# Three edits to a one-core attention, MLP and soft-expert kernel: two GEMM-1 blocks ahead of a data check, VectorE's first chunks in another order, and the last softmax in another order with filler matmuls

## The chip, the cores and the metric

The kernel runs on one core of a Trainium2 chip, as one launch. The metric is the time of the execution on the device in microseconds (us); lower is better. The time before is the median of three runs.

## The reference

Three layers in fp32. The first is a linear attention with a decay per feature, over 4 batches, 8 heads, 768 steps and head size 48. The second is an MLP on the 3072 x 384 result, with w_in (384 x 2048), a sigmoid gelu and w_out (2048 x 384). The third is a soft mixture of 8 experts with 4 slots each, d_ff 1024.

```python
for t in range(S):                      # attention
    cur = einsum('bhd,bhe->bhde', u[None] * kt, vt)
    y[:, :, t] = einsum('bhd,bhde->bhe', rt, state + cur)
    state = wt[:, :, :, None] * state + einsum('bhd,bhe->bhde', kt, vt)
h = x @ w_in                            # MLP
x = (h * (1.0 / (1.0 + exp(-1.702 * h)))) @ w_out
logits = x @ phi                        # 32 slots
d = softmax of logits over the 3072 tokens;  slot_input = d.T @ x
slot_out[e] = maximum(slot_input[e] @ w1[e], 0.0) @ w2[e]
c = softmax of logits over the 32 slots;     out = c @ slot_out
```

## The kernel before, in words

**Tiles and stages.** The sequence is cut into 24 chunks of 128 steps (`NCH`), and one chunk holds all eight heads of a batch. The MLP works in nine steps (`SIZES` = 2, 2, 2, 3, 3, 3, 3, 3, 3 chunks). In a step, GEMM-1 runs in 16 blocks of 128 hidden features (`F` counts the blocks over all steps, 0 to 143), each nine matmuls: every fp32 operand is split into a high and a low fp32r part, and three products are summed (xh·wi_hi, xl·wi_hi, xh·wi_lo). ScalarE takes the gelu of a block (L747) and rounds it to its high part (L751, `gh`). VectorE makes the low part (L1053, `gl`), and TensorE adds the block into GEMM-2 (L1241) two blocks later.

**What sets the order.** Each engine's program is written out by hand and walks one list, `slots_of_work`. An entry holds a block F, perhaps one of four pieces (j = 0 to 3) of a chunk's attention that this block hosts, perhaps a piece of the soft-expert softmax of the step before, and perhaps a job on the output softmax. Engines meet only at semaphores, so an instruction that waits holds all that stands behind it on its engine. In the first MLP step the attention of chunks 2 and 3 is hosted by blocks (2, 3, 5, 6) and (8, 9, 11, 12).

**The prologue.** Chunks 0 and 1 (`PRE` = 2) have no MLP work to host them. On VectorE `start_up()` (L966 to L1019) orders their pieces: `decays` and `invert` are scans over 516 elements; `decayed` and `grown_keys` make r and k for the score matmuls; `bonus` forms r·u·k by four instructions for each chunk (L867); `mask_scores`, `bonus_values` (bonus times v), `first_state` and `next_state` (the 48 x 48 states), `add_output`. On TensorE a chunk is `score` (L1145), four transposes (L1259), the bonus matmul (L1268), `gather_state` (L1156), `output` (L1165, L1171). TensorE then brings both outputs into the MLP's layout (`permute`, L1202, six fp32 matmuls of 128 columns each), ScalarE rounds them (`xh`, L794) and VectorE makes `xl` (L491). Between these stand matmuls on a zero tile (`keep_warm`, L1196).

**The data check.** The fast attention holds only if all decays lie in 0.625 to 1.5. Six slabs of 1536 columns are tested: slabs 0 to 2 on ScalarE (`test_decays`, L731 and L733), slabs 3 to 5 on VectorE (`bound_decays`, L963 and L964) and TensorE, which sums their bounds (L1304, L1306). A one-element matmul (L1312) and two VectorE instructions (L1003, L1004) give the flag. TensorE, VectorE and SyncE read it and branch. With these inputs the slow branch is not taken. Before, all of the MLP stands behind the branch.

**Weights.** w_in and w_out come in four slabs each through two staging buffers. ScalarE makes a slab's high part (`high_part`, L725), VectorE its low part (`low_part`, L1024), and only then does GpSimd issue the load of the slab after next. Counted through, even numbers are w_in, odd ones w_out.

**The tail.** After the last MLP step: three turns of x2 (L1352), logits (L1363), their maxima (L1100 to L1103), the exponentials (L817 to L819), the turn of e and l (L1370), the maximum over the three row groups (`common`, L1336 to L1338), `merge` (the normalised shares, with L1342), `add` (L1375, L1130), the slot inputs (L1384), ScalarE's copy `siT` (L465), and then the experts' first layer (L1394), relu (L462, L497), turns (L1406), second layer (L1425), and the output (L1450).

The lines on which the timing turns, in order: what VectorE does between the branch and the first blocks, how GEMM-2 waits, and the test's place on ScalarE.

```python
for j in range(4):
    front_part(PRE, j)      # decays, bonus, invert, decayed, grown_keys of chunk 2
low_part(1)
...
pe.wait_ge(gl_done, F - 1)  # GEMM-2 of block F - 2
...
early = {(0, 0): [(test_decays, 0)], (1, 0): [(high_part, 0), (test_decays, 1)],
         (1, 1): [(test_decays, 2)], (1, 3): [(high_part, 1)]}
```

## Time and profile before

| | |
|---|---|
| median of 3 runs | 626.76 us (626.35 to 627.07) |
| the profiled execution | 626.53 us, of which its span 624.8 us |
| mean granted TensorE clock | 0.978 |
| TensorE (PE) busy | 591.9 us, 95% of the span |
| VectorE (DVE) busy | 332.4 us, 53% |
| ScalarE (ACT) busy | 263.3 us, 42% |
| GpSimd (POOL) busy | 12.3 us, 2% |

The span is what the profile covers; the time of the execution is 1.73 us longer. The rows further below come from four views. The chain of waits is followed back from the last instruction, step by step, to what released it. The timeline lists instructions in order of time. The windows give the busy time of each engine in a stretch. The list of DMA issues gives size and time to landing. Overlapping instructions on TensorE are modelled, so a busy TensorE may still be a slow one: its granted clock (PEclk, 1.00 for 2.4 GHz and 0.50 for 1.2 GHz) stands beside it.

### The profile page before, as it was taken

How to read it: one execution, taken by the hardware profiler on the slowest of the kernel's cores; microseconds unless marked ns; L12 is line 12 of the kernel's file. 1: busy time of each engine (PE TensorE's matmuls, PEld its weight loads, DVE VectorE, ACT ScalarE, POOL GpSimd, SP SyncE). 2: the span in 40 equal slices, each digit the busy share in tenths (PEclk: the TensorE clock that was granted, in tenths of full speed). 3: DMA queues.
4: the chain of work that ended last, by engine and by line, in shares of the span. 5: the costliest groups of instructions: out<-in, count | busy, mean ns of one | idle time of the engine just before them, and what ended most of it. 6: DMA issues, size and time to landing. Idle time of an engine off the chain costs nothing.

```text
span 624.8 us, 15049 instructions
## 1 busy us (share of the span) xinstructions
PE 591.9 (95%) x6291; PEld 522.6 (84%) x6291; DVE 332.4 (53%) x730; ACT 263.3 (42%) x535; POOL 12.3 (2%) x30
## 2 busy tenths in 40 slices
PE   6969989999999999999999999999999999997983
PEld 4749889889989998999999989999999999995332
DVE  6879845648836662666356635664455324223214
ACT  3624634364353335433543354335433446453214
POOL 4001000000000000000000000000000000000000
PEclk9998999999999999999999999999999999998896
DMA  8937613204513331233123321233030196766528
GB/s 295 357 98 216 194 41 100 78 22 108 150 39 86 88 88 36 60 99 99 39 60 99 83 56 38 73 89 98 2 100 26 35 378 228 248 231 221 204 100 302
DMA packets 46309, 77.48 MB, mean 124 GB/s; under 512 B 3297, under 2 KB 35041, under 8 KB 43665
## 3 DMA queue, kind: packets, MB, share of 16 engines
q1 hardware_dynamic: 45040, 71.80, 37.1%
q0 software_dynamic: 1200, 4.72, 2.5%
q8 instruction: 50, 0.82, 0.6%
q14 instruction: 19, 0.15, 0.1%
HBM read 67.46 MB, written 9.04 MB: 122 GB/s over the span
## 4 chain that ended last, share of the span: by engine, by line
PE 90%; DVE 5%; issue 2%; POOL 1%; ACT 1%; DMA 1%; DVEq 0%; POOLq 0%; ACTq 0%
PE hps L1226 32%; PE acc L1241 32%; PE yps L1165 2%; PE mps L1259 2%; PE acc L1394 2%; PE zps L1145 2%; PE mps L1352 2%; PE zps L1165 2%; PE zps L1156 1%; PE zps L1171 1%; PE mps L1375 1%; PE mps L1363 1%; PE acc L1196 1%; PE mps L1425 1%; PE hps L1425 1%
## 5 line engine op out<-in xcount | busy, mean ns | idle before, releaser
L1053 DVE TENSOR_TENSOR gl<-g,gh 128x384 fp32r<-128x384 f32 (+1 forms) x144 | 73.9, 514 | 232.5 <-ACT gh L751 232.3
L1226 PE MATMUL hps<-xh,wi_hi 128*128 128x384 f32 (+1 forms) x432 | 147.2, 341 | 3.0 <-DVE xl L491 1.6
L1226 PE MATMUL hps<-xh,wi_lo 128*128 128x384 f32 (+1 forms) x432 | 137.2, 318 | 0.0
L1226 PE MATMUL hps<-xl,wi_hi 128*128 128x384 f32 (+1 forms) x432 | 137.1, 317 | 0.0
L1241 PE MATMUL acc<-wo_hi,gh 128*128 128x384 f32 x384 | 130.0, 338 | 4.2 <-DVE gl L1053 3.8
L1241 PE MATMUL acc<-wo_hi,gl 128*128 128x384 f32 x384 | 129.6, 338 | 0.0
L1241 PE MATMUL acc<-wo_lo,gh 128*128 128x384 f32 x384 | 129.6, 337 | 0.0
L747 ACT ACTIVATE g<-hps 128x384 f32<-128x384 f32 (+1 forms) x144 | 65.6, 456 | 142.0 <-PE hps L1226 138.4
L751 ACT ACTIVATE gh<-g 128x384 fp32r<-128x384 f32 (+1 forms) x144 | 70.4, 489 | 129.2 <-PE acc L1241 128.7
L1226 PEld LDWEIGHTS hps<-xh,wi_hi 128*128 128x128 f32 x432 | 81.4, 188 | 13.2 <-issue 8.3
L1226 PEld LDWEIGHTS hps<-xl,wi_hi 128*128 128x128 f32 x432 | 81.7, 189 | 0.9
L1226 PEld LDWEIGHTS hps<-xh,wi_lo 128*128 128x128 f32 x432 | 81.4, 188 | 0.0
L1241 PEld LDWEIGHTS acc<-wo_hi,gh 128*128 128x128 f32 x384 | 72.4, 188 | 5.5 <-DVE gl L1053 4.7
L1241 PEld LDWEIGHTS acc<-wo_lo,gh 128*128 128x128 f32 x384 | 72.5, 189 | 0.0
L1241 PEld LDWEIGHTS acc<-wo_hi,gl 128*128 128x128 f32 x384 | 72.4, 189 | 0.0
L860 DVE TENSOR_TENSOR_SCAN decay<-raw,restart 112x516 f32<-112x516 f32 x24 | 29.4, 1227 | 2.9 <-issue 1.6
L1165 PEld LDWEIGHTS yps<-rp,midway 48*48 48x48 f32 x384 | 22.9, 120 | 9.0 <-issue 5.2
L879 DVE TENSOR_TENSOR_SCAN inv<-raw,ends 112x516 f32<-112x516 f32 x24 | 29.6, 1234 | 0.8
L1165 PE MATMUL yps<-rp,midway 48*48 48x64 f32 x384 | 26.3, 218 | 2.9 <-DVE midway L931 2.8
L867 DVE SCALAR_TENSOR_TENSOR ruk<-raw,ucols 112x128 f32<-112x128 f32 x96 | 28.3, 337 | 0.0
L1165 PE MATMUL zps<-rp,state 48*48 48x64 f32 x384 | 25.9, 218 | 0.0
L1165 PEld LDWEIGHTS zps<-rp,state 48*48 48x48 f32 x384 | 22.4, 120 | 0.0
(225 smaller groups left out, 733.6 us busy)
## 6 DMA issues: line engine op xcount, KB each, us to landing
raw<-dmaj SPq DMA_DIRECT2D x23, 903.0 KB, 5.7
w1s<-w SPq DMA_DIRECT2D x16, 768.0 KB, 6.8
w2s<-w SPq DMA_DIRECT2D x16, 768.0 KB, 7.2
vn<-vnat SPq DMA_DIRECT2D x24, 192.0 KB, 2.5
tests<-wall SPq DMA_DIRECT2D x6, 768.0 KB, 14.0
out<-obuf SPq DMA_DIRECT2D x12, 384.0 KB, 4.1
y_scratch<-ybuf SPq DMA_DIRECT2D x44, 96.0 KB, 2.0
x<-y_scratch SPq DMA_DIRECT2D x22, 192.0 KB, 2.5
```

The lines of the kernel that those rows point to most:

```text
L747: act.activation(g32[F % 2][:, 0:wide], hps[F % 2][:, 0:wide], ACT.Gelu_apprx_sigmoid).then_inc(gelu_done, 1)
L751: act.activation(gh[F % 2][:, 0:wide], g32[F % 2][:, 0:wide], ACT.Copy).then_inc(gh_done, 1)
L860: dve.tensor_tensor_scan(flat[0], flat[1], flat[2], 1.0, ALU.mult, ALU.max).then_inc(scanned, 1)
L867: last = dve.scalar_tensor_tensor(ruk[n % 2][:, p, :], field(n, RR)[:, p], ucols[:, p:p + 1], field(n, KK)[:, p], ALU.mult, ALU.mult)
L879: dve.tensor_tensor_scan(flat[0][:, ::-1], later, flat[1][:, ::-1], 1.0, ALU.mult, ALU.add).then_inc(inverted, 1)
L1053: dve.tensor_tensor(out=gl[F % 2][:, 0:wide], in0=g32[F % 2][:, 0:wide], in1=gh[F % 2][:, 0:wide].bitcast(fp32), op=ALU.subtract).then_inc ...
L1145: last = pe.matmul(score_banks(n)[par][cols, p * HALF:(p + 1) * HALF], kd[n % 2][rows, p, cols], rp[n % 2][rows, p, cols], start=True, sto ...
L1165: return pe.matmul((zps, yps)[c][rows, p * HALF:(p + 1) * HALF], (state[n % 2], midway)[c][rows, p, :], rp[n % 2][rows, p, HALF * c:HALF * ...
L1226: last = pe.matmul(hps[F % 2][:, 0:wide], w[:, g, at:at + 128], v[i % 2][:, g, 0:wide], start=m == 0, stop=m == len(terms) - 1)
L1241: last = pe.matmul(acc[m][:, 0:DM], a[k][:, rows], w[:, f % CW, :], start=f == 0 and w is hi and a is gh, stop=f == NF - 1 and a is gl)
L1259: last = pe.transpose(mps[:, p * R:(p + 1) * R], kd[n % 2][:, p, :], ident[0:R, 0:R])
L1352: last = pe.transpose(ps[:, g * 128:(g + 1) * 128], x2[:, m, g * 128:(g + 1) * 128], ident[:, :])
```

## The change

**Prologue, checks.** ScalarE now tests four slabs (0, 1, 2, 4) and VectorE two (3, 5). ScalarE tests two of its four after it has made both `xh`. TensorE sums the bounds in pieces of 256 columns instead of 512.

**Prologue, GEMM-1.** Blocks 0 and 1 of GEMM-1 run ahead of the flag, between the sums. ScalarE's gelu of block 0 waits for `settled`, which one matmul behind TensorE's branch sets. On the slow branch both blocks are computed again.

**Prologue, order.** u is multiplied into four small head matrices (`heads_u`, by ScalarE), so that VectorE forms r·k in one instruction (`products`) and the bonus is four matmuls of 128 columns instead of one of 512. VectorE's pieces of chunks 0 and 1 stand in another order, `permute(0)` goes in front of `output(1)`, and chunk 2's front parts move from before `low_part(1)` to behind `gl` of blocks 0 and 1. In the first step the attention of chunks 2 and 3 is hosted by blocks (3, 4, 5, 6) and (8, 9, 10, 11). The load of phi is issued later.

**Tail.** For the last step only: e is turned before the maxima are combined, l is turned apart and later, and `add` comes before `merge`. The slot inputs are formed with unnormalised shares. The normaliser (one matmul against 128 columns, then `shares`) is applied as the scale of the experts' relu. Behind five groups of this stretch TensorE runs 2 to 4 fp32 matmuls of the identity with itself (`keep_ready`), 14 in all.

```diff
-TP, TA = 6, 3
+TP = 6
+ON_ACT, ON_DVE = (0, 1, 2, 4), (3, 5)
...
-SPAN = 512
+SPAN = 256
...
-                chunks = hosts[SIZES[i + 1]] if i else ((2, 3, 5, 6), (8, 9, 11, 12))
+                chunks = hosts[SIZES[i + 1]] if i else ((3, 4, 5, 6), (8, 9, 10, 11))
...
-                          for g in ("turn0", "turn1", "turn2", "logits", "common", "turn_e", "merge", "add")]
+                          for g in ("turn0", "turn1", "turn2", "logits", "turn_e", "common", "add", "merge")]
...
-                act.activation(hid[q][:, 0:512], (acc[0], acc[2])[q][:, :], ACT.Relu).then_inc(hid_act, 1)
+                act.wait_ge(merge_done, 1)
+                act.activation(hid[q][:, 0:512], (acc[0], acc[2])[q][:, :], ACT.Relu, scale=shares[:, 1:2]).then_inc(hid_act, 1)
...
-                dve.tensor_scalar(hid[q][:, 512:1024], (acc[1], hps[0])[q][:, :], 0.0, None, ALU.max).then_inc(hid_dve, 1)
+                dve.tensor_scalar(hid[q][:, 512:1024], (acc[1], hps[0])[q][:, :], shares[:, 1:2], 0.0, ALU.mult, ALU.max).then_inc(hid_dve, 1)
...
-            sp.dma_start(phis[:, :, :], phi.rearrange("(g p) s -> p g s", p=128)).then_inc(phi_in, 16)
...
+                    sp.dma_start(phis[:, :, :], phi.rearrange("(g p) s -> p g s", p=128)).then_inc(phi_in, 16)
                     sp.wait_ge(flag_made, 1)
...
+            def high_first(c):
+                act.wait_ge(permuted, c + 1)
+                act.activation(xh[0][:, :, c * C:(c + 1) * C], permuted_x(c), ACT.Copy).then_inc(xh_done, 1)
             early = {(0, 0): [(test_decays, 0)], (1, 0): [(high_part, 0), (test_decays, 1)],
-                     (1, 1): [(test_decays, 2)], (1, 3): [(high_part, 1)]}
+                     (1, 3): [(high_first, 0), (high_first, 1), (test_decays, 2), (test_decays, 3), (high_part, 1)]}
...
+            act.wait_ge(headsum_made, 1)
+            act.wait_ge(u_in, 16)
+            for p in range(HP):
+                last = act.activation(heads_u[:, p, :], headsum_f[:, :], ACT.Copy, scale=ucols[:, p:p + 1])
+            last.then_inc(heads_made, 1)
...
+                    if F == 0:
+                        act.wait_ge(settled, 1)
...
-                if F is None and attn == (PRE - 1, 3):
-                    for c in range(PRE):
-                        act.wait_ge(permuted, c + 1)
-                        act.activation(xh[0][:, :, c * C:(c + 1) * C], permuted_x(c), ACT.Copy).then_inc(xh_done, 1)
...
+                        act.wait_ge(l_turned, 1)
+                        act.activation(logits[:, BASE[i]:BASE[i] + SIZES[i], :],
+                                       acc[2][:, 0:NG].rearrange("t (a s) -> t a s", s=NS),
+                                       ACT.Copy).then_inc(el_done, 1)
...
+                        if i == NST - 1:
+                            act.activation(el[:, 0:wide], zps[:, 0:wide], ACT.Copy).then_inc(el_last, 1)
+                            continue
...
+            def products(n):
+                dve.tensor_tensor(out=ruk[n % 2][:, :, :], in0=field(n, RR), in1=field(n, KK), op=ALU.mult).then_inc(ruk_made, 1)
...
-                bonus(0, 0)
-                bonus(0, 1)
+                products(0)
+                dve.wait_ge(made, CONSTANTS)
+                for m in range(3):
+                    rows = slice(m * NS, (m + 1) * NS)
+                    dve.tensor_copy(fold[rows], ident[rows, rows])
                 decays(1)
-                dve.wait_ge(made, CONSTANTS)
                 mask_scores(0)
-                bonus_values(0)
                 invert(1)
+                decayed(1)
+                grown_keys(1)
                 first_state(0)
                 next_state(0)
-                decayed(1)
-                grown_keys(1)
-                bonus(1, 0)
+                bonus_values(0)
+                products(1)
                 add_output(0)
-                bonus(1, 1)
                 mask_scores(1)
                 bonus_values(1)
                 first_state(1)
                 next_state(1)
-                for m in range(3):
-                    rows = slice(m * NS, (m + 1) * NS)
-                    dve.tensor_copy(fold[rows], ident[rows, rows])
-                bound_decays(TA)
                 add_output(1)
                 low_part(0)
                 rest_x(dve, 0, 0)
                 rest_x(dve, 0, 1)
-                dve.wait_ge(tested, TA)
-                dve.tensor_reduce(outsum[:, :], outside[:, 0:TA], AX, ALU.add).then_inc(flag_sum, 1)
-                for k in range(TA + 1, TP):
-                    bound_decays(k)
+                for j in range(len(ON_DVE)):
+                    bound_decays(j)
+                dve.wait_ge(tested, len(ON_ACT))
+                dve.tensor_reduce(outsum[:, :], outside[:, :], AX, ALU.add).then_inc(flag_sum, 1)
...
-                for j in range(4):
-                    front_part(PRE, j)
...
+                if F in (0, 1):
+                    front_part(PRE, 2 * F)
+                    front_part(PRE, 2 * F + 1)
...
+                        dve.wait_ge(beta_done, 1)
+                        dve.tensor_scalar(merge[:, :, :], fold[:, :].unsqueeze(1).broadcast_to([NG, 4, NS]), beta[:, :], None,
+                                          ALU.mult).then_inc(den_weighted, 1)
...
-                        dve.wait_ge(beta_done, 1)
-                        dve.wait_ge(den_done, NST)
-                        chain(dve.tensor_scalar(merge[:, 0, :], fold[:, :], beta[:, :], None, ALU.mult))
-                        dve.tensor_scalar(merge[:, 1, :], merge[:, 0, :], den[:, NST % 2:NST % 2 + 1], None,
-                                          ALU.mult).then_inc(den_weighted, 1)
                         dve.wait_ge(den_merged, 1)
-                        chain(dve.tensor_scalar(merge[:, 2, :], zps[0:NG, 0:NS], 1e-9, None, ALU.add))
-                        chain(dve.reciprocal(merge[:, 2, :], merge[:, 2, :]))
-                        dve.tensor_tensor(out=merge[:, 1, :], in0=merge[:, 0, :], in1=merge[:, 2, :],
-                                          op=ALU.mult).then_inc(merge_done, 1)
+                        chain(dve.tensor_scalar(shares[:, 0:1], yps[:, 0:1], 1e-9, None, ALU.add))
+                        dve.reciprocal(shares[:, 1:2], shares[:, 0:1]).then_inc(merge_done, 1)
...
+            def keep_ready(times):
+                for _ in range(times):
+                    pe.matmul(hps[1][:, 0:128], ident[:, :], ident[:, :], start=True, stop=True)
...
+                        pe.wait_ge(heads_made, 1)
                         pe.wait_ge(ruk_made, n + 1)
-                        pe.matmul(bonus_bank(n)[0:R, :], headsum_f[:, :], ruk[n % 2][:, :, :].rearrange("d p t -> d (p t)"),
-                                  start=True, stop=True).then_inc(u_done, 1)
+                        for p in range(HP):
+                            last = pe.matmul(bonus_bank(n)[0:R, p * C:(p + 1) * C], heads_u[:, p, :], ruk[n % 2][:, p, :],
+                                             start=True, stop=True)
+                        last.then_inc(u_done, 1)
...
+                if F is None and attn == (PRE - 1, 2):
+                    pe.wait_ge(y_done, 1)
+                    pe.wait_ge(scored, 2 * PRE)
+                    permute(0, permuted)
                 if F is None and attn == (PRE - 1, 3):
-                    for c in range(PRE):
-                        pe.wait_ge(y_done, c + 1)
-                        permute(c, permuted)
-                        keep_warm(WARM)
+                    pe.wait_ge(y_done, PRE)
+                    permute(1, permuted)
+                    keep_warm(WARM)
+                    pe.wait_ge(xl_done, PRE)
+                    pe.wait_ge(lo_done, 1)
+                    hidden_layer(0).then_inc(h_done, 1)
                     pe.wait_ge(ones_made, 1)
-                    for k in range(TA, TP):
-                        pe.wait_ge(bounded_done, k - TA + 1)
...
-                        last.then_inc(bounds_summed, 1)
-                        if k + 1 < TP:
-                            keep_warm(WARM)
+                    sum_bounds(0)
+                    hidden_layer(1).then_inc(h_done, 1)
+                    sum_bounds(1)
                     pe.wait_ge(flag_sum, 1)
...
+                    pe.matmul(acc[0][:, 0:256], warm[:, 0:128], warm[:, 128:384], start=True, stop=True).then_inc(settled, 1)
...
+                    elif what == "turn_e" and i == NST - 1:
+                        pe.wait_ge(et_done, NST)
...
+                        pe.wait_ge(e_done, NST)
+                        pe.transpose(acc[2][:, 0:NG], lT[:, :], ident[0:NG, 0:NG]).then_inc(l_turned, 1)
                     if what == "merge":
+                        pe.wait_ge(gathered_done, NST)
                         pe.wait_ge(den_weighted, 1)
-                        pe.matmul(zps[0:NG, 0:NS], ones_sq[:, :], merge[:, 1, :], start=True, stop=True).then_inc(den_merged, 1)
+                        for g in range(G):
+                            last = pe.matmul(mps[:, g * NS:(g + 1) * NS], gathered[:, g * 128:(g + 1) * 128], merge[:, 0, :],
+                                             start=True, stop=True)
+                        last.then_inc(si_psum, 1)
+                        pe.wait_ge(den_done, NST)
+                        pe.matmul(yps[:, 0:1], merge[:, :, :].rearrange("r a s -> r (a s)"), den[:, NST % 2:NST % 2 + 1],
+                                  start=True, stop=True).then_inc(den_merged, 1)
+                        keep_ready(3)
...
+                        if ends and m == 2:
+                            keep_ready(3)
...
+                        if i == NST - 1:
+                            pe.transpose(zps[:, 0:wide], eT[0:wide, :], ident[0:wide, 0:wide]).then_inc(e_turned, 1)
+                            keep_ready(2)
...
-            pe.wait_ge(*mps_read)
-            pe.wait_ge(gathered_done, NST)
-            pe.wait_ge(merge_done, 1)
-            for g in range(G):
-                last = pe.matmul(mps[:, g * NS:(g + 1) * NS], gathered[:, g * 128:(g + 1) * 128], merge[:, 1, :],
-                                 start=True, stop=True)
-            last.then_inc(si_psum, 1)
```

On VectorE, from the flag to the first score mask of chunk 2, the order before is the following. `wo_lo` and `wi_lo` are the low parts of weight slabs, `gl` those of MLP blocks, `decay`, `ruk`, `inv`, `rp`, `kd` chunk 2's front parts.

```order
L860 SCALAR_TENSOR_TENSOR decay_71<-raw_67,restart 112x516
L867 SCALAR_TENSOR_TENSOR ruk_79<-raw_67,ucols 112x128 x2
L875 RECIPROCAL ends<-decay_71 112x4
L879 SCALAR_TENSOR_TENSOR inv<-raw_67,ends 112x516
L867 SCALAR_TENSOR_TENSOR ruk_79<-raw_67,ucols 112x128 x2
L885 TENSOR_TENSOR rp_75<-raw_67,decay_71 112x512
L890 TENSOR_TENSOR kd_77<-raw_67,inv 112x512
L1024 TENSOR_TENSOR wo_lo_58<-stage_119,wo_hi_57 128x1536
L1053 TENSOR_TENSOR gl_110<-g_0_105,gh_107 128x256
L1024 TENSOR_TENSOR wi_lo_52<-stage_118,wi_hi_51 128x1536
L1053 TENSOR_TENSOR gl_111<-g_1_106,gh_108 128x256
L1053 TENSOR_TENSOR gl_110<-g_0_105,gh_107 128x256
```

In the changed kernel the same place on VectorE reads:

```order
L1048 TENSOR_TENSOR wo_lo_58<-stage_120,wo_hi_57 128x1536
L1076 TENSOR_TENSOR gl_111<-g_0_106,gh_108 128x256
L884 SCALAR_TENSOR_TENSOR decay_71<-raw_67,restart 112x516
L891 SCALAR_TENSOR_TENSOR ruk_79<-raw_67,ucols 112x128 x2
L903 RECIPROCAL ends<-decay_71 112x4
L907 SCALAR_TENSOR_TENSOR inv<-raw_67,ends 112x516
L891 SCALAR_TENSOR_TENSOR ruk_79<-raw_67,ucols 112x128 x2
L1048 TENSOR_TENSOR wi_lo_52<-stage_119,wi_hi_51 128x1536
L1076 TENSOR_TENSOR gl_112<-g_1_107,gh_109 128x256
L913 TENSOR_TENSOR rp_75<-raw_67,decay_71 112x512
L918 TENSOR_TENSOR kd_77<-raw_67,inv 112x512
L1076 TENSOR_TENSOR gl_111<-g_0_106,gh_108 128x256
```

The low part of the w_out slab and of block 0 now come first, and `kd` of chunk 2 stands behind four more instructions than it did.

On TensorE, the tail from the last logits to the first expert matmul reads before:

```order
L1363 MATMUL mps<-x2t,phis 32x128 x9
L1336 MATMUL yps<-ident,top 1x96
L1338 MATMUL yps<-ones,common 96x1
L1370 MATMUL mps<-ident,eT 128x96
L1370 MATMUL mps<-ident,lT 128x96
L1342 MATMUL zps<-merge,ones_sq 96x32
L1375 MATMUL mps<-x_112,el 32x384 x3
L1384 MATMUL mps<-merge,gathered 128x32 x3
```

and after, where `hps<-ident` rows are the fillers:

```order
L1422 MATMUL mps<-x2t,phis 32x128 x9
L1218 MATMUL hps<-ident 128x128 x4
L1431 MATMUL zps<-ident,eT 128x96
L1218 MATMUL hps<-ident 128x128 x2
L1383 MATMUL yps<-ident,top 1x96
L1385 MATMUL yps<-ones,common 96x1
L1388 MATMUL acc<-ident,lT 128x96
L1442 MATMUL mps<-x_113,el 32x384 x3
L1218 MATMUL hps<-ident 128x128 x2
L1393 MATMUL mps<-merge,gathered 128x32 x3
L1397 MATMUL yps<-den,merge 128x1
L1218 MATMUL hps<-ident 128x128 x3
```

The turn of e stands ahead of the maxima now, the normaliser's matmul behind the slot inputs, and fillers stand between, three of them directly ahead of the experts.

## Rows read from the trace of the kernel before

**Rows 1.** Page, the chain that ended last: its shares by engine.

```profile
PE 90%; DVE 5%; issue 2%; POOL 1%; ACT 1%; DMA 1%; DVEq 0%; POOLq 0%; ACTq 0%
```

**Rows 2.** Chain of waits, prologue and first step: start us, us, what.

```profile
26.66 1.34 PE hps L1202 x12
...
37.34 0.15 DVE flag L1004
...
45.96 2.29 PE acc L1241 x6
...
88.42 1.33 PE hps L1226 x9
```

**Rows 3.** Timeline, VectorE: start us, us, instruction, [idle before <-releaser].

```profile
25.96 0.95 DVE L964 TENSOR_SCALAR bounded<-tests 128x1536 fp32r<-128x1536 f32 x1
...
36.63 0.68 DVE L1003 TENSOR_REDUCE insum<-acc 1x1 f32<-1x512 f32 x1 [2.04 <-PE acc L1312]
...
39.10 1.23 DVE L860 TENSOR_TENSOR_SCAN decay<-raw,restart 112x516 f32<-112x516 f32 x1 [1.62 <-issue]
...
48.80 0.43 DVE L1053 TENSOR_TENSOR gl<-g,gh 128x256 fp32r<-128x256 f32 x1 [0.89 <-ACT gh L751]
...
65.43 1.76 DVE L1024 TENSOR_TENSOR wo_lo<-stage,wo_hi 128x1536 fp32r<-128x1536 f32 x1 [2.87 <-ACT wo_hi L725]
...
80.76 0.41 DVE L954 TENSOR_TENSOR ybuf<-yps,ybuf 112x256 f32<-112x256 f32 x1
```

**Rows 4.** Timeline, ScalarE, 25 to 64 us.

```profile
25.61 1.56 ACT L731 ACTIVATE tests<-tests,test_bias 128x1536 f32<-128x1536 f32 x1
...
28.68 0.18 ACT L733 ACTIVATION_READ_ACCUMULATOR tests<-tests,test_bias 128x1 f32 x1
...
29.96 0.49 ACT L794 ACTIVATE xh<-hps 128x384 fp32r<-128x384 f32 x1 [0.72 <-PE hps L1202]
...
40.11 0.39 ACT L747 ACTIVATE g<-hps 128x256 f32<-128x256 f32 x1 [8.28 <-PE hps L1226]
...
63.91 1.49 ACT L725 ACTIVATE wo_hi<-stage 128x1536 fp32r<-128x1536 f32 x1 [3.15 <-DMA stage<-w_out]
```

**Rows 5.** Timeline, TensorE, 17 to 20 us.

```profile
17.03 0.22 PE L1165 MATMUL yps<-rp,midway 48*48 48x64 f32 x1 [0.95 <-DVE midway L931]
...
19.92 0.60 PE L1259 MATMUL mps<-ident,kd 112*128 112x112 f32 x4
```

**Rows 6.** DMA issues of 45 to 46.5 us: median us to landing last.

```profile
stage<-w_out POOLq DMA_DIRECT2D x1, 768.0 KB, 5.0
```

**Rows 7.** DMA issues of 54 to 55 us.

```profile
stage<-w_out POOLq DMA_DIRECT2D x1, 768.0 KB, 9.4
```

**Rows 8.** Windows: stretch, length, busy us of PE, PEld, DVE, ACT, POOL, PEclk, DMA, GB/s.

```profile
44.00:46.00 2.00, 0.04 (x1) 0.04 (x1) 2.00 (x3) 0.00 (x0) 0.12 (x1) 0.57 0.00 0
...
573.00:574.00 1.00, 0.54 (x5) 0.48 (x8) 0.37 (x2) 0.25 (x2) 0.00 (x0) 0.67 0.87 326
...
583.00:584.00 1.00, 1.00 (x12) 0.32 (x8) 0.00 (x0) 0.60 (x1) 0.00 (x0) 0.71 0.00 0
```

**Rows 9.** Chain of waits, tail: start us, us, what.

```profile
560.56 0.78 PE mps L1375 x6
...
569.63 0.89 PE mps L1363 x18
...
571.33 0.26 PE yps L1336
...
573.99 1.47 PE mps L1375 x6
...
576.19 1.47 PE mps L1384 x6
...
577.99 8.11 PE acc L1394 x48
...
586.53 2.71 PE acc L1394 x24
```

More of the change, by code:

```diff
@@ L129, in attention_mlp_soft_experts @@
             xl[i] = sb(f"xl{i}", [128, G, ST], f32r)
+        heads_u = sb("heads_u", [R, HP, R], at=place[0])
         g32 = [sb(f"g32_{i}", [128, ST]) for i in range(2)]
@@ L862, in bonus @@
             def bonus(n, half):
-                if n == 0 and half == 0:
+                if n == PRE and half == 0:
                     dve.wait_ge(u_in, 16)
@@ L1322, in _ @@
                         pe.wait_ge(split_again, PRE)
+                        for F0 in range(2):
+                            hidden_layer(F0)
+                    pe.matmul(acc[0][:, 0:256], warm[:, 0:128], warm[:, 128:384], start=True, stop=True).then_inc(settled, 1)
                 if job is not None and job != "exps":
```

105 lines of the change are left out of this document (61 added, 44 removed).

## The prediction

> **What bounds the kernel now.** I read the chain of waits first. TensorE carries 90% of it, VectorE 5% [rows 1], so most of the span is matmul work that the change leaves alone. What can move are the places where TensorE isn't the bound, and the chain has two: the prologue with the first MLP step, and the tail between the last MLP block and the experts.
>
> In the prologue the flag is started at 37.34, and TensorE's next link of weight is GEMM-2 of block 0 at 45.96 [rows 2]. Between them stand VectorE's branch (1.62 us of "issue"), chunk 2's front parts from 39.10, and `low_part(1)`; ScalarE had its first gelu at 40.11 [rows 3, 4]. From 39.10 to the end of chunk 3's output (80.76 + 0.41 = 81.2) VectorE waits only twice for any length: 0.89 us for a gelu and 2.87 us for ScalarE, which itself waited 3.15 us for a w_out slab [rows 3, 4]. So the stretch is VectorE's, and the first block of the second step starts at 88.42 [rows 2]. In the windows the granted clock falls to the lower level (1.2 GHz) in 44 to 46, after TensorE stood idle [rows 8].
>
> In the tail the chain hops between engines from 569.63 to 577.99 [rows 9]. The clock falls in 573 to 574 (mean 0.67) and is back in 583 to 584 (0.71) [rows 8]: it is low from about 573.3 to 583.4, 10.1 us.
>
> **The change part by part: up to the flag.** (1) VectorE's order. TensorE waited 0.95 us for `midway` of chunk 0 at 17.03 [rows 5], because the scan `inv` stood ahead of it. Now the state comes as soon as its matmuls are through, and chunk 1 starts up to 0.95 us earlier; I take 0.75, since `keep_warm` matmuls stand in the gap. (2) `permute(0)` (1.34 us [rows 2]) moves ahead of `output(1)` and stays on the path, but the group of `keep_warm` behind it goes: about 0.6. The second `xh` was at 29.96 [rows 4]; 29.96 - 0.75 - 0.6 = 28.6, over at 29.1.
>
> (3) The bonus is four matmuls of 128 columns with a load each, in place of one of 512. Four transposes with four loads took 0.60 [rows 5], and a `permute` matmul of 128 columns 1.34 / 6 = 0.22. So the split costs between 0 and 0.9 a chunk; I take 0.1, the row with four loads. The Trainium skill (TensorE: Matmul & The Clock Gate, section Step-by-step: what each phase is for) says that weight loads are pulled ahead of running matmuls; by that the split costs nothing, and the sum would be 0.1 better. (4) `heads_u` is four small copies on ScalarE, and `products` one instruction for four on VectorE: both lie beside the wait for GpSimd's constants.
>
> (5) The tests. A slab took ScalarE from 25.61 to 28.86, and 3.17 where one follows another [rows 4]. Two now stand behind the second `xh`: 29.1 + 6.35 = 35.45. VectorE's two slabs are at most four times 0.95 [rows 3] behind `xl`, about 33.5, and TensorE, with two GEMM-1 blocks and 24 short sums in between, also comes out near 35.3: all three engines meet. With the sum of 0.15 and the one-element matmul the reduction starts near 35.8, not 36.63, and takes 256 elements in place of 512: near 0.42 (a 256-column instruction on VectorE takes that [rows 3]) instead of 0.68. The flag comes 0.85 + 0.25 = **1.1 us earlier**. No idle slot is left on ScalarE there: what it is late, the flag is late.
>
> (6) The load of phi, now issued at about 27 us, isn't needed before the second step: nothing.
>
> **From the flag to block 16.** The branch costs what it cost (1.62). `low_part(1)` and `gl` of block 0 are done at 39.6 and 40.0 instead of 45.6 and 45.9, because 4.8 us of front parts stand behind them now, and because ScalarE has its gelu at about 38.0, right behind `settled`, not at 40.11. But VectorE has the same instructions in both orders, and it is the bound, so the gain isn't these 6 us. It is the flag's 1.1, plus what VectorE no longer waits. Of 3.76 us (0.89 + 2.87) I count:
> - GpSimd loads a slab when `low_part` of the slab before it in its buffer is done. `low_part(1)` six us earlier starts slab 3 at 40. Alone it takes 5.0 [rows 6], and VectorE reaches `low_part(3)` at about 47. It ends at 48.8 instead of 54.2, and slab 5, issued at 49, takes 9.4 at worst [rows 7]. It is there at 58.5, and VectorE, by its own queue, gets to `low_part(5)` at 60.7. The 2.87 goes.
> - The 0.89 goes too, since gelu and `gh` of block 2 are done at about 41.8.
> - What is late next: near 63 VectorE waits for TensorE's block 7 and 8, which can't run faster than about 2.1 us a block. I make that wait 1.65.
>
> So 3.76 - 1.65 = 2.1, and **the first step ends 1.1 + 2.1 = 3.2 us earlier**: block 16 at 85.2 instead of 88.4. TensorE's own idle stretch (42.2 to 45.6, for `gl` of block 1, behind the scans) stays, and so, I expect, does the fall of its clock in it. This costs little, since VectorE is the bound there. Later steps run as before.
>
> **The tail.** What the low level costs is in the rows: `add` takes 1.47 against 0.78 for the same six records at full clock, the slot inputs 1.47 (0.78 by the same ratio), and the first 48 expert matmuls 8.11 against 2 x 2.71 [rows 9]: 0.69 + 0.69 + 2.69 = 4.1 us.
>
> A filler is an fp32 matmul of 128 columns: 0.22 by `permute` [rows 2], 0.15 by the transposes [rows 5]. I take 0.22, the plain matmul. The Trainium skill (TensorE: Matmul & The Clock Gate, section Terms) gives fp32 a transpose mode four times as fast, by which the transposes' row would make a filler 0.60, and the tail 2.4 us longer than I sum. The `permute` row speaks against that.
>
> With the clock kept: four fillers behind the logits end at 571.4, under the wait for the exponential; e is turned at 571.8; two fillers later TensorE turns the maxima at 572.4, not 571.33 (+1.1). Maxima, spread and the turn of l take it to 573.8, `add` to 574.6, VectorE's accumulation to 575.3, the slot inputs to 576.05, the normaliser's matmul and three fillers to 577.0. Experts start at 577.0, not 577.99: -1.0. (ScalarE's `siT`, 0.3, lies under the fillers; the two fillers behind `add` under VectorE.) With 2.69 for the experts, **the tail is 3.7 us shorter**. The scale in the relu costs nothing: `shares` are ready two us before.
>
> **Sum.** 626.53 - 3.2 - 3.7 = 619.6 for the profiled execution. The median lies 0.2 above its time: **619.9 us**.
>
> **Rivals.**
> - *A: the clock isn't kept in the tail* (624.3). For it: it fell in the middle of small matmuls, at one waiting about 0.6 to 0.8 us at each hop, and hops stay. Against it: TensorE would be occupied some 80% of 569.6 to 577, where now it is half of that. Then `add` and the slot inputs lose 1.4, the last four small groups and fillers about 1.0, and the experts start at 579.4; if the clock is back at 583.4 as now, they lose 2.0. End of these 24 + 24 matmuls: 586.8, against 586.1 now: +0.7, so 626.53 - 3.2 + 0.7 + 0.2.
> - *B: the slabs still set the first step* (622.0). VectorE's 2.87 stays, or another wait takes its place, if slab 3 takes 9.4 as slab 5 did, since its high part stands ahead of a gelu on ScalarE. Then only the flag's 1.1 is left: 626.53 - 1.1 - 3.7 + 0.2. For it: 9.4 [rows 7]; against it: 5.0 when alone [rows 6], and nothing else is loaded at 40.
> - *C, slower: TensorE's clock doesn't come back in the first step* (629.8). It falls in the idle stretch before 45.6, and the work behind it is broken up by waits for VectorE. A microsecond of dense work at the lower level costs half a microsecond (8.11 against 5.42 [rows 9]). If it stays low for 20 us more than now, that is +10, and 619.9 + 9.9 = 629.8. It decides from 14 us (6.9 / 0.5). Against it: the same dip is there now, and ends within seven us.
> - *D: nothing to be seen* (626.8): ScalarE's tests come so late that the flag isn't earlier, and the fillers eat what the clock gives back.
>
> **How the numbers follow.** The forecast has 0.60, A 0.14, B 0.16, C 0.05, D 0.05. A and B are faster too, so faster by over 0.2% (1.25 us, about what a measurement of this kernel tells from no change) has 0.90, within it 0.05, slower 0.05. The open costs are the bonus (up to 0.8 more a chunk), the fillers (0.5 less to 2.4 more) and VectorE's waits (2.1 less to 1.7 more). The range takes in A and B, and leaves out C, D and the far ends: 618.0 to 624.6.
>
> **What would show it.** In the profile after: the flag near 36.2, first gelu near 38.0, GEMM-2 of block 0 near 40.1; no wait of ScalarE for a w_out slab near 60; block 16 near 85.2. In the tail, PEclk 1.00 throughout, `add` near 0.8, and the first 48 expert matmuls in 5.4. Wrong: a flag at 37 or later; VectorE waiting over 2 us for a high part; PEclk 0.50 behind the logits; a last block of the first step that starts no earlier than before.

## The result, and the profile after

| kernel | median, us | executions | range | ratio to before, 95% interval |
|---|---|---|---|---|
| before | 627.0 | 80 (all jobs) | 623.8 to 630.3 | |
| changed | 623.65 | 7 | 620.3 to 625.8 | 0.9947, 0.9921 to 0.9973 |
| changed, all three jobs | 622.1 | 19 | 620.1 to 625.8 | 0.9947, 0.9910 and 0.9920 |

A job is one session in which executions of the changed kernel and of the kernel before were timed side by side. The change makes the kernel faster, by 3.1 us in the first job and by 4.9 over all executions. I had forecast 6.9. The executions of the changed kernel spread over 5.7 us, so 1.5 of the 3.8 us missing in the first job is its median's place in that spread. The profiled execution took 622.08, its span 620.4 against 624.8: 4.4 less. The page's shares of the chain are like those of before [rows 1]:

```profile
PE 88%; DVE 5%; issue 2%; DMA 2%; POOL 1%; ACT 1%; DVEq 0%; SPq 0%; POOLq 0%; ACTq 0%
```

The chain of waits in the prologue and the first step answers to [rows 2] (start us, us, what):

```profile
12.60 1.71 PE acc L1311 x8
...
22.34 0.47 issue
...
37.26 0.15 DVE flag L1030
...
46.62 2.29 PE acc L1283 x6
...
53.78 0.43 ACT gh L771
...
80.22 3.39 DMA y_scratch<-ybuf
...
83.77 2.44 DMA x<-y_scratch
...
```

The flag (the instruction on VectorE that ends the data check) starts 0.08 us earlier than before, where I had put 1.1. GEMM-2 of block 1 (2.29 for its six matmuls) runs at the lower clock, which I call half clock below. A piece called `issue` on TensorE is a rest for which the profile shows no cause. The end of the first step is no longer a matmul chain but chunk 3's way through memory: its store, then the load of x.

VectorE's timeline answers to [rows 3]:

```profile
36.81 0.41 DVE L1029 TENSOR_REDUCE insum<-acc 1x1 f32<-1x256 f32 x1 [0.28 <-PE acc L1354]
...
38.95 1.76 DVE L1048 TENSOR_TENSOR wo_lo<-stage,wo_hi 128x1536 fp32r<-128x1536 f32 x1 [1.55 <-issue]
...
54.24 0.43 DVE L1076 TENSOR_TENSOR gl<-g,gh 128x256 fp32r<-128x256 f32 x1 [1.20 <-ACT gh L771]
...
66.40 0.42 DVE L1076 TENSOR_TENSOR gl<-g,gh 128x256 fp32r<-128x256 f32 x1 [1.68 <-ACT gh L771]
```

The reduction over 256 elements takes 0.41 (0.68 before), as forecast. The waits of 2.87 and 0.89 are gone and 1.68 has come near 66 (I had 1.65), but 1.20 at 54.24 is new: the `gh` it waits for hangs on GEMM-1's block 4, which TensorE ran at half clock. ScalarE's timeline, with [rows 4]:

```profile
25.54 0.49 ACT L747 ACTIVATE xh<-hps 128x384 fp32r<-128x384 f32 x1 [0.31 <-PE hps L1253]
29.50 0.49 ACT L747 ACTIVATE xh<-hps 128x384 fp32r<-128x384 f32 x1 [3.48 <-PE hps L1253]
...
39.29 0.38 ACT L767 ACTIVATE g<-hps 128x256 f32<-128x256 f32 x1 [1.58 <-PE acc L1367]
```

The second `xh` comes at 29.50 instead of my 28.6, and ScalarE stands idle for 3.48 us ahead of it. The windows, with [rows 8] (stretch, length, busy time of PE, PEld, DVE, ACT, POOL, PEclk, DMA share, GB/s):

```profile
9.00:16.00 7.00, 6.57 (x87) 6.14 (x88) 5.19 (x11) 3.67 (x4) 0.24 (x2) 0.59 1.03 408
...
44.00:52.00 8.00, 5.38 (x48) 4.83 (x49) 8.00 (x14) 3.23 (x5) 1.51 (x2) 0.59 0.54 179
84.00:92.00 8.00, 6.05 (x72) 5.42 (x71) 3.00 (x8) 3.20 (x8) 0.00 (x0) 1.00 0.08 25
560.00:577.00 17.00, 16.06 (x125) 13.09 (x126) 6.49 (x19) 6.08 (x17) 0.00 (x0) 1.00 0.69 234
577.00:600.00 23.00, 22.98 (x228) 8.22 (x224) 4.60 (x9) 4.86 (x9) 0.00 (x0) 1.00 0.60 207
```

From 9 to 16 us the clock is at the lower level (mean 0.59). For the profiled execution of before the same window shows 1.00, but the durations there say otherwise. Set beside e9, the kernel before with a longer warm-up (below), its first matmuls take as long as at half clock. In the chain of before, and then in that of e9:

```profile
9.84 1.13 PE hps L1145 x32
10.97 0.94 PE mps L1259 x4
...
13.00 1.22 PE acc L1268 x2
```

```profile
9.67 0.69 PE hps L1145 x32
10.37 0.53 PE mps L1259 x4
...
11.50 0.87 PE acc L1268 x2
```

The changed kernel's first two groups are the same as before's (1.13 and 0.94). Half clock lasted to about 13.7 in before's execution (0.35 us more than 0.87 is some 0.7 us at half clock) and to 14.7 here. So both profiles have the half clock in the prologue, here for one us more. The tail's chain, with [rows 9]:

```profile
567.91 0.67 PE hps L1218 x6
568.58 0.87 PE mps L1422 x18
571.05 0.47 PE hps L1218 x4
572.78 0.81 PE mps L1442 x6
...
574.28 0.85 PE mps L1393 x6
575.33 0.78 PE hps L1218 x6
576.11 5.29 PE acc L1455 x48
```

The groups `hps L1218` are the fillers. `add` takes 0.81 instead of 1.47, the slot inputs 0.85 instead of 1.47, the first 48 expert matmuls 5.29 instead of 8.11. Block 16 started 1.0 us earlier than before, the outputs' first matmul 4.47 (604.17 against 608.64): the tail gave about 3.4 of the 4.4 us, prologue and first step 1.0.

### The profile page after: what moved, and what is told of

The parts are those of the page before. It is cut to its first block, busy times and chain, and to the rows that moved or that the text cites. A ratio compares the mean times of both kernels' runs of the same rounds, so it can differ in the third digit from the quotient of the medians.

```text
span 620.4 us, 15118 instructions
## 1 busy us (share of the span) xinstructions
PE 589.9 (95%) x6326; PEld 527.6 (85%) x6326; DVE 329.1 (53%) x719; ACT 267.9 (43%) x542; POOL 12.6 (2%) x30
## 4 chain that ended last, share of the span: by engine, by line
PE 88%; DVE 5%; issue 2%; DMA 2%; POOL 1%; ACT 1%; DVEq 0%; SPq 0%; POOLq 0%; ACTq 0%
PE hps L1233 32%; PE acc L1283 31%; PE yps L1187 2%; PE mps L1301 2%; PE zps L1167 2%; PE mps L1409 2%; PE zps L1178 2%; PE zps L1187 2%; PE zps L1193 1%; PE acc L1455 1%; PE mps L1422 1%; PE mps L1442 1%; PE hps L1486 1%; PE acc L1223 1%; PE mps L1486 1%
## 5 line engine op out<-in xcount | busy, mean ns | idle before, releaser
L891 DVE SCALAR_TENSOR_TENSOR ruk<-raw,ucols 112x128 f32<-112x128 f32 x88 | 25.9, 336 | 0.0
```

Source lines behind the costliest of these rows:

```text
L891: last = dve.scalar_tensor_tensor(ruk[n % 2][:, p, :], field(n, RR)[:, p], ucols[:, p:p + 1], field(n, KK)[:, p], ALU.mult, ALU.mult)
```

## The experiments

Each was timed in five rounds beside the kernel before. The runs e5a to e8a have the edits and expectations of e5 to e8, which gave no time. Line numbers are those of the kernel in question. "Flag" is the start of that instruction on VectorE, "block 16" that of the second step's first matmul, both in the profiled execution, as is the span. Bonus(0) is the bonus matmul of chunk 0. All times are in us.

| run | median (n) | ratio, 95% | flag | block 16 | span |
|---|---|---|---|---|---|
| before | | | 37.34 | 88.42 | 624.8 |
| changed | 623.65 (7) | 0.9921 to 0.9973 | 37.26 | 87.40 | 620.4 |
| e4 changed again | 621.17 (6) | 0.9883 to 0.9936 | 35.65 | 84.93 | 619.5 |
| e12 changed, third | 622.05 (6) | 0.9900 to 0.9939 | 36.26 | 86.79 | 619.9 |
| e1 tail alone | 624.85 (12) | 0.9944 to 0.9973 | 37.67 | 90.48 | 623.8 |
| e2 front alone | 625.80 (12) | 0.9960 to 0.9991 | 37.38 | 87.93 | 624.3 |
| e3 no fillers in the tail | 624.54 (10) | 0.9936 to 0.9968 | 36.95 | 85.83 | 623.2 |
| e5a test between | 620.92 (7) | 0.9879 to 0.9941 | 35.92 | 84.95 | 621.4 |
| e6a rests filled | 619.39 (6) | 0.9850 to 0.9909 | 35.24 | 83.70 | 617.0 |
| e7a longer warm-up | 620.36 (6) | 0.9854 to 0.9915 | 35.29 | 84.16 | 618.9 |
| e13 the same again | 620.83 (6) | 0.9888 to 0.9945 | 35.10 | 83.54 | 616.6 |
| e14 first step's rests | 620.85 (6) | 0.9871 to 0.9913 | 37.65 | 86.33 | 619.8 |
| e8a blocks behind flag | 623.98 (12) | 0.9930 to 0.9973 | 36.06 | 87.54 | 620.6 |
| e9 before, longer warm-up | 626.45 (12) | 0.9970 to 1.0000 | 37.84 | 88.87 | 623.8 |
| e10 e5a and e6a | 619.57 (5) | 0.9846 to 0.9889 | 38.53 | 86.97 | 619.9 |
| e11 and chunk 3 earlier | 619.32 (5) | 0.9859 to 0.9900 | 34.34 | 82.78 | 615.6 |

**The two halves.** e1 has only the tail's hunks of the diff, e2 only the others.

> The kernel before with the tail's part of the change alone (order of the last step's softmax, row sums merged into the experts' scale, filler matmuls). Theory 1 (the two parts of the change add up; the tail gave 3.4 of the 4.4 us by which the span shrank): 626.8 - 3.4 = 623.4, ratio 0.9946, the 48 first expert matmuls in 5.3 to 5.5 us and the block at slot 16 still at 88.4. Theory 2 (the parts depend on each other, because the clock in the tail follows what the whole kernel did before): 625 to 627.

> The prologue's part of the change alone, with the tail of the kernel before. Theory 1: 626.8 - 1.0 = 625.8, ratio 0.9984, block 16 at 87.4, the expert matmuls 8.1 us again. Rival (the prologue's part is worth nothing by itself and its 1.0 us is one execution's scatter): 626.8. What I had predicted for it was 623.6.

The tail alone gives 2.1 us (ratio 0.9959), the front alone 1.2 (0.9975); together 3.3 by the medians and 4.1 by the ratios, the whole change 4.9 by the medians of all jobs: as well as these intervals can tell, they add up. Of my two terms the front's 3.2 is far off, and the tail's 3.7 lies just outside e1's interval (1.7 to 3.5). One profile can mislead here: up to block 16, e1 does the work of before, and in its profile block 16 comes 2.06 us later than in that of before, with the rest of the span 3.06 shorter.

**The tail's fillers.** e3:

```
             def keep_ready(times):
-                for _ in range(times):
-                    pe.matmul(hps[1][:, 0:128], ident[:, :], ident[:, :], start=True, stop=True)
+                for _ in range(0):
+                    pass
```

> The changed kernel without its 14 filler matmuls in the tail; all else of the tail's reordering stays. Theory 1 (the fillers keep the granted clock at 1.00 there, as the reordering alone does not): the clock falls in the tail, the 48 first expert matmuls take 8.1 instead of 5.3 us, the six adds 1.47 instead of 0.81, time 623.65 + 3.2 = 626.8. Rival (the shorter chain between the matmuls keeps the clock by itself): 623.3 to 623.7, since the fillers cost at most 0.3.

2.4 us slower than the changed kernel (622.1), where I had expected 3.2. The clock falls to a mean of 0.84 in 560 to 577, and the chain has the low-clock durations back:

```profile
572.51 1.47 PE mps L1442 x6
...
576.53 7.97 PE acc L1455 x48
```

So the fillers are what keeps the clock. From e2 (old tail) to e3 the reordering alone gives 1.3 us, from e3 to the changed kernel the fillers 2.4. They don't keep it every time: of twelve profiled kernels with fillers, two (e5a and e7a) show means of 0.92 and 0.90 in 560 to 577, and e7a's 48 expert matmuls took 6.13.

**The changed kernel again** (e4, e12).

> The changed kernel once more, unchanged, to see which differences between the two profiled executions come back. Theory 1: median 623.0 to 624.3, ratio 0.9947; in the profile the flag at 37.3, gelu(0) at 39.3, the idle 1.2 us of VectorE before the difference of tile 4, block 16 at 87.4, the experts' 48 matmuls in 5.3. Rival (the first step's 1.0 us is scatter): block 16 anywhere from 86.5 to 88.4, and the median elsewhere with it.

> The changed kernel a third time, beside the next two on one chip. Theory 1 (its time is the sum of a fixed part and of stretches at half clock and fetch rests in the prologue, which differ from execution to execution): median 622.3, executions from 620 to 626, span minus the flag's start 583.1 to 583.9 as in its two profiles.

The two profiles of one kernel, e4 here beside the one above, differ by 1.6 us at the flag. In e4 the chain and the windows read:

```profile
12.56 1.12 PE acc L1311 x8
...
84.93 2.29 PE hps L1233 x9
```

```profile
9.00:16.00 7.00, 6.43 (x99) 5.70 (x101) 5.97 (x14) 3.68 (x4) 0.24 (x2) 0.76 1.04 408
...
44.00:52.00 8.00, 6.66 (x71) 5.94 (x72) 8.00 (x15) 5.73 (x9) 1.51 (x2) 1.00 0.48 165
84.00:92.00 8.00, 7.07 (x67) 6.73 (x68) 3.32 (x7) 2.54 (x6) 0.00 (x0) 0.79 0.00 0
```

By the windows the low clock ended near 13.0 instead of 14.7, bonus(0) took 1.12 instead of 1.71, and there was no `issue` rest of 0.47 at 22.3. TensorE's rest before GEMM-2's block 1 was nearly as long (2.71 against 3.15) and the clock stayed at 1.00 behind it; it fell in the rest before block 16 instead (2.42 us), whose matmuls then took 2.29 instead of 1.31. So where the half clock falls changes from one execution to the next, and not by the length of the last rest alone: in e12 it fell ahead of GEMM-2's block 1 too, behind rests of only 1.53 and 1.37. In e12 the span less the flag's start is 583.6, close to the other two (583.1 and 583.9): what the flag is late, the end is late.

**Filling TensorE's rests** (e6a all three, e7a and e13 the warm-up, e14 the first step's two).

```
-WARM_UP = (512,) * 8
+WARM_UP = (512,) * 18
...
+                    if F == NF:
+                        pe.wait_ge(y_done, BASE[2])
+                        keep_busy(8)
...
+                    if F == 3:
+                        keep_busy(12)
                     pe.wait_ge(gl_done, F - 1)
```

> The changed kernel with matmuls on zeros in three rests of TensorE: 10 more of 512 columns in the warm-up (it rests there from 5.2 to 9.4), 12 of 256 columns ahead of GEMM-2's block 1 (rest 43.5 to 46.6) and 8 ahead of block 16 (rest 85.2 to 87.4). Theory 1 (the missing 2 us and the scatter of 5.7 us between executions are stretches at half clock that follow these rests): granted clock 1.00 from 2 to 95 us, bonus(0) in 1.12 instead of 1.71 us, GEMM-2 block 1 in 1.05 instead of 2.29, time 622.3 - 0.9 (prologue) - 1.0 (first step) = 620.4 and the spread under 3 us. Rival (half clock comes back in another rest, or the fillers push the work behind them): 622 to 623.

> The changed kernel with the longer warm-up alone (18 matmuls of 512 columns instead of 8). Theory 1: clock 1.00 from 9.4 to 15 us, flag 0.9 us earlier than in executions at half clock there (37.3 to 36.4 or less), time 622.3 - 0.9 = 621.4; the first step's own stretch at half clock stays. Rival (the constants or the loads of v set the start of the prologue and nothing is gained): 622.3.

> The changed kernel with the longer warm-up alone, again (18 matmuls of 512 columns instead of 8). Theory 1 (half clock in the prologue costs the changed kernel 1.5 to 2 us and cost the kernel before 0.3 to 0.7): 620.4, ratio 0.988 to 0.990, that is 1.9 under the changed kernel. Rival (the 1.9 us between 620.36 and 622.27 came from different chips and sessions): the same median as the changed kernel in this job, within 0.5.

> The changed kernel with the fillers in the first step alone (12 ahead of GEMM-2's block 1, 8 ahead of block 16), the warm-up as it was. Theory 1 (the first step's half clock costs 1.0, whether it falls on GEMM-2's block 1 or on block 16): 622.3 - 1.0 = 621.3, flag as in the changed kernel, block 16 within 48.5 us of the flag instead of 49.3 to 50.1. Rival (the clock of the first step follows from the prologue's, and without the longer warm-up the fillers do nothing): 622.3.

By the medians the warm-up is worth 1.5 us (12 executions, median 620.6, against 19 of the changed kernel, 622.1), the first step's fillers 1.3, all three 2.7. The scatter of the times isn't gone with it: 1.9 us over e6a's six executions, but 7.3 over e13's six and 4.0 over the five each of e10 and e11, so those stretches of half clock aren't its only source. In the direct comparison of e12 and e13 the warm-up gave 1.2, with overlapping intervals, so its size is known to perhaps one us; the flag is better evidence. With the clock at 1.00 from 9 to 16 us it starts at 35.10 to 35.29, in three profiles out of three; with bonus(0) at half clock (1.59 to 1.71) it starts at 36.3 to 37.7, in five (changed, e2, e3, e12, e14). In e14 the flag is late, and block 16 still comes 48.7 us behind it. But that isn't shown to be the fillers' work: in its profile the half clock fell at 40 to 44, ahead of them, as it did in e3, which has no such fillers and 48.9. Their worth rests on the times, whose intervals overlap with the changed kernel's. The windows of e13:

```profile
9.00:16.00 7.00, 5.44 (x121) 4.79 (x124) 6.44 (x15) 3.79 (x4) 0.24 (x2) 1.00 1.03 407
38.00:44.00 6.00, 4.56 (x23) 3.85 (x21) 5.97 (x11) 3.03 (x6) 0.77 (x1) 0.72 0.47 140
44.00:52.00 8.00, 7.21 (x74) 6.32 (x74) 7.97 (x17) 5.65 (x9) 1.51 (x2) 1.00 0.57 191
```

My expectation for e6a, 1.00 throughout, was wrong. The clock falls in 38 to 44 there too (0.77), with all three rests filled, as it does here in e13: soon after TensorE's rest at the branch (1.25). It costs little at that place, since block 16 follows the flag by 48.4 to 48.5 in both.

**The same warm-up in the kernel before** (e9; the same edit of `WARM_UP`).

> The kernel before with the longer warm-up alone. Theory 1 (before the change TensorE had slack in the prologue, so its half clock cost little there: flag at 37.67 with it in the run with the tail's edits, 37.34 without; the change took the slack away, so that the same half clock costs 1.2 to 2 us): flag at 37.3, time 626.8 - 0.3 = 626.5, ratio 0.9995. Rival (the half clock costs both kernels alike, and the profiled execution of before had merely escaped it): ratio 0.997, as the changed kernel gained 1.9 us of its 622.3 by this warm-up.

The ratio is 0.9985 (0.9970 to 1.0000): 0.7 us, between the two theories' 0.3 and 1.9. The flag doesn't come earlier at all: 37.84, with bonus(0) in 0.87, against 37.67 in e1, where it took 1.71. Theory 1 would explain that by TensorE's slack in the prologue (the 0.95 of [rows 5]), which would have taken up the half clock. The chain of e9 speaks against it:

```profile
16.73 0.78 PE acc L1196 x4
...
25.11 1.34 PE hps L1202 x12
...
28.27 1.95 issue
30.21 0.28 PE hps L1202
```

TensorE still waits 0.94 for `midway`, and yet it is 1.8 us ahead of before's profile at the first of these rows (18.57 there) and 1.55 ahead at `permute(0)` (26.66). The slack had hidden little of the half clock. The lead went in a rest of 1.95 in the middle of `permute(1)`, which before's profile doesn't have. Without it, by my estimate (30.52 - 1.95), the second `xh` would have started at about 28.6, which is 1.4 ahead of before's. The changed kernel, for its part, waits for `midway` again when its clock is up (1.1 us in e6a, e7a and e13), and its chunk 1 starts no earlier than e9's: 17.41 to 17.59 against 17.44. So the half clock reaches `permute` in both kernels. Whether the kernel before gains less from the warm-up than the changed one stays open: the interval of e9 goes from 0 to 1.9 us and holds both theories.

**The flag earlier** (e5a).

```
-  (1, 3): [(high_first, 0), (high_first, 1), (test_decays, 2), ...
+  (1, 3): [(high_first, 0), (test_decays, 2), (high_first, 1), ...
...
                     sum_bounds(0)
-                    hidden_layer(1).then_inc(h_done, 1)
                     sum_bounds(1)
...
                               skip_group_check=True).then_inc(flag_psum, 1)
-                    keep_warm(WARM)
+                    hidden_layer(1).then_inc(h_done, 1)
```

> The changed kernel with ScalarE's third decay test between the two rounded copies of x (in the 3.48 us in which ScalarE idles there) and GEMM-1's block 1 behind the flag's sums on TensorE. Theory 1 (the flag waits for the four tests and for TensorE's sums, which end together): both end 1.1 us earlier, flag at 36.1 instead of 37.3 in an execution with the same clock, block 16 as much earlier, time 622.3 (the changed kernel's median over both sessions) - 1.1 = 621.2. Rival (a first step that is set by VectorE's chain from flag to chunk 3 keeps nothing of it, since slabs and x loads keep their own dates): 622.3. Second rival: the test delays the second rounded copy and with it VectorE's remainder by 0.2 to 0.5, and the flag gains only 0.6.

Flag at 35.92 with bonus(0) at half clock (1.71), 1.2 under the five profiles' mean of 37.1; time 1.2 under 622.1. The tests ended 2.8 us earlier (`outsum` at 33.59 against 36.37), and TensorE's sums alone set the flag now, by a wait of 1.74. Theory 1 holds in size; its interval alone (0.9879 to 0.9941) wouldn't exclude nothing.

**GEMM-1's two blocks back behind the branch** (e8a).

```
                     sum_bounds(0)
-                    hidden_layer(1).then_inc(h_done, 1)
+                    keep_warm(WARM)
...
+                    for F0 in range(2):
+                        hidden_layer(F0).then_inc(h_done, 1)
```

> The changed kernel with GEMM-1's blocks 0 and 1 back behind the branch (filler matmuls in their place between the sums). Theory 1 (gelu(0) then waits 1.06 us more for block 0, and VectorE, which sets the first step, waits as long for the first gl): gelu(0) 1.0 us later, block 16 0.8 to 1.0 later, time 622.3 + 0.9 = 623.2. Rival (VectorE's remainder of the slab covers it, or the x load at the step's end does): 622.3 with block 16 where it was.

1.9 slower than the changed kernel; block 16 comes 51.5 us behind the flag instead of 49.3 to 50.5 in the changed kernel's three profiles. More than the 1.06 of one block: TensorE also stood longer at the branch, and the blocks ran in part at half clock. Chain of e8a:

```profile
36.36 3.21 issue
39.57 0.39 PE acc L1362
39.95 1.63 PE hps L1233 x9
```

In the changed kernel that rest is 1.25. Whether the longer one belongs to this order or to this execution, one profile can't say.

**Both together, and chunk 3 a block earlier** (e10, e11).

```
-  ((3, 4, 5, 6), (8, 9, 10, 11))
+  ((3, 4, 5, 6), (7, 8, 9, 10))
```

> The changed kernel with the test between the rounded copies, block 1 behind the sums and all three rests filled. Theory 1 (both gains add: the rests gave 2.9 us, the flag 1.35): flag at 34.2, block 16 at 82.6, time 619.4 - 1.1 = 618.3. Rival (at full clock the flag is no longer set by the tests but by what comes before them, or the slabs' loads set the first step): 619.4.

> The same with chunk 3 hosted in blocks 7 to 10 instead of 8 to 11, so that its store and the load of x that block 16 waits for start a block earlier. Theory 1 (VectorE and not the hosting sets when chunk 3's output is added; the rest before block 16 is 0.63 us with the fillers): 618.3 - 0.3 = 618.0. Rival (the work lands on blocks where VectorE is full already and the GEMM chain waits for it): 618.6 to 619.

Neither is told from e6a (619.4, 619.6, 619.3), though e11's flag at 34.34 is 0.8 to 1.0 under those of e6a, e7a and e13. All three beat the changed kernel; e6a and e11 are 7.6 and 7.7 us under before's median over all jobs. e10's profiled execution shows what else moves the flag, with the clock at 1.00 throughout. Its chain:

```profile
2.20 9.34 DMA raw<-dmaj
...
21.28 1.54 issue
...
29.62 0.80 issue
```

The load of chunk 1 (7.3 us in e11's execution) took 9.3, VectorE's scan started at 11.56 instead of 10.01, and TensorE stood for 1.54 and 0.80 in the middle of its own matmuls. That is 3.9 of the 4.2 us between the two flags, and the spans differ by 4.3.

## Why the prediction was half right

The forecast was 6.9 in three terms. The changed kernel has three profiles (changed, e4, e12); set against the one of before they give this:

| stretch | forecast | changed, e4, e12 | mean |
|---|---|---|---|
| up to the flag | 1.1 | 0.08, 1.69, 1.08 | 0.95 |
| flag to block 16 | 2.1 | 0.94, 1.80, 0.55 | 1.1 |
| block 16 to the end | 3.7 | 3.4, 1.8, 3.3 | 2.8 |

The means add up to 4.9, like the medians. About 1.0 of the missing 2.0 us is the first step's, 0.9 lies behind block 16.

**(1) to (5), the flag 1.1 us earlier.** Right on the mean of three profiles, and wrong in the first one, in which the flag at 37.26 was my own sign of being wrong. The step that failed there is the one number for the second `xh`, "29.96 - 0.75 - 0.6 = 28.6": it came at 29.50, 27.89 and 28.51. In the first profile TensorE rested for 0.47 at 22.3, and half clock lasted one us longer than in before's, which is worth half a us. From the second `xh` to the flag it took 7.75 in all three, against my 7.6. That the mean fits is partly luck: I read before's durations as full clock, while half clock stands in them up to about 13.7, and one term of 1.1 can't be told from executions that differ by 1.6. How much the new order gives at the same clock stays open. With half clock past chunk 0, e14's flag (37.65) is no earlier than e1's (37.67).

**(3) The bonus split** costs nothing: 1.71 (x8) against 1.71 (x2) for chunk 0 at half clock (e2, e1), 0.88 against 0.86 for chunk 1 at full clock. I had 0.1 with a bound of 0.9. The Trainium skill (TensorE: Matmul & The Clock Gate, section Step-by-step: what each phase is for) has weight loads pulled ahead of running matmuls; these rows agree.

**(5) The three engines meet:** they did, some 1.1 us later than I had put it. `outsum` waited for the tests and ended at 36.5, TensorE's last sum at 36.6.

**First step, 2.1 us beyond the flag.** This is the term that failed on the mean. The slab waits behaved as forecast. What failed is the sentence on the dip, that is on the stretch at half clock: "This costs little, since VectorE is the bound there." From flag to block 16 I had forecast 49.0 us (85.2 - 36.2), where before took 51.1. It is 48.4 to 49.3 in the profiles in which the clock was up in 44 to 52 (e3, e4, e6a, e13, e14, e10 and e11; in e7a and e5a nearly, 0.86 and 0.79), e8a apart, whose blocks stand elsewhere. It is 50.1 to 50.6 where the clock was down there (changed, e2, e12). Half clock at that place delays GEMM-1's block 4, and VectorE then waits for a `gh` with its whole queue behind it: 1.20 in the changed kernel, 1.34 in e12, nothing in e4, e3 and e14. So 1.1 to 1.6 of the 2.1 go back, in executions where the dip falls there. A wait of 0.38 at 64.30, which I hadn't counted, adds to it.

**The tail, 3.7.** Near where the clock was up: 3.4 in the profile, 3.7 from e2 to the changed kernel, with each duration as forecast (`add` 0.81, experts 5.29, a filler 0.67 / 3 = 0.22 for my 0.22). From before to e1 it was 2.1. Part of what is missing there isn't the tail's: in e4 block 16 itself ran at half clock (2.29 for its nine matmuls, against 1.31), and 1.8 is left behind block 16. Rival A, the clock not kept, is e3, and happens in some executions with fillers too. How often it does, and so its share of the median, isn't known.

**Rivals.** B's 622.0 is the changed kernel's median over all jobs, by luck and another mechanism: the slabs were in time. C named the right place and the wrong size; the clock was back after some seven us, as before the change. For A I had read the clock of before as back at 583.4; by the window's mean of 0.71 it is 583.6, which changes A by 0.1.

**The sum.** 619.9 lies just under the fastest of the changed kernel's 19 executions (620.1). The sum took each term at its best and the half clock in the first step at nothing. That e6a, with the rests filled, takes 619.4 is near the forecast, but it is another kernel and doesn't confirm the sum.

## What to carry to other kernels

Check the granted clock of a profiled execution by the durations of the same instruction early and late, before taking durations from it: a window that said 1.00 held matmuls of 1.13 that take 0.69 at full clock. Where a clock dip falls decides its price. The same dip cost little behind the branch and 1.1 to 1.6 us some six us later, so "the other engine is the bound" isn't a reason to price it at nothing. With executions that differ by 1.6 us at one flag, a term of 1 us needs more than one profile on either side. A few matmuls on zeros in TensorE's rests gave 2.7 us here, the whole reordering of the front 1.2 to 1.6.

## What the runs showed of the hardware

- The same kernel's clock falls at different places in different executions: after rests of TensorE of 2.7 and 3.2 us at one place it stayed up once and fell once, it fell there once more after rests of 1.5 and 1.4, and it fell once after 2.4 us elsewhere. The Trainium skill (TensorE: Matmul & The Clock Gate, Part 1: The HAM clock gate) says that the warm-up at a kernel's start varies from run to run of one kernel. The three profiles of the changed kernel agree: half clock ended near 14.7, 13.0 and 14.1 us.
- The same section of the Trainium skill puts the cost of the warm-up at under 1% of a typical span and advises against fitting a model to it. The runs agree on the size: the longer warm-up gave 1.5 of 622 us, 0.2%. But that is nearly a third of the 4.9 us that the change gained, so for predicting a change it counts.
- The clock's records can be missing: in before, e5a and e12 the window of 9 to 16 us shows 1.00, though bonus(0) took 1.22, 1.71 and 1.59 there against 0.87 at full clock (e9). All ten profiles with the unaltered warm-up have 1.09 to 1.14 for chunk 0's first group of matmuls, against 0.69 in e9. The durations decide.
- TensorE rests of 0.4 to 1.95 us for which the profile shows no cause ("issue") stand in the middle of a group of matmuls in some executions (changed 0.47 near 22, e10 1.54 near 21 and 0.80 near 30, e9 0.39 near 21 and 1.95 near 28) and are missing in others (e4). In the changed kernel's profile a 0.02 MB packet of the instruction queue moved at 20.0 to 20.5, in e4's at 17.5 to 18, and in that of before, which has no such rest there, at 20.5 to 21. So a late packet alone doesn't make a rest, and no run shows what does.
